# Attention, expert layer and gated layer on one core: the skipped TensorE code in loops, the tile table in two parts, w2's last pieces split in their own tile

## What is computed

```
state = f[t] * state + outer(k[t], v[t]);  y[t] = q[t] @ state      # B=4, H=8, S=768, D=48; f = sigmoid(f_logit)
x = y as 3072 tokens of 384
logits = x @ w_gate + modality_bias[modality_id];  e = argmax(logits)      # 8 experts
x = softmax(logits)[e] * (relu(x @ w1[e]) @ w2[e])                         # w1 384x1024, w2 1024x384
xn = x / sqrt(mean(x*x) + 1e-6) * rms_g
out = (silu(xn @ w_gate2) * (xn @ w_val)) @ w_out                          # 384x1536, 1536x384
```

## Time and profile before

| what | value |
|---|---|
| median of 3 runs | 838.8 us |
| lowest and highest | 836.85 and 844.91 us |
| the profiled execution | 838.23 us, span 836.5 us, mean TensorE clock 0.994 |
| TensorE matmuls | 811.1 us busy (97%) |
| TensorE weight loads | 737.0 us busy (88%) |
| VectorE | 452.0 us busy (54%) |
| ScalarE | 380.0 us busy (45%) |
| GpSimd | 140.5 us busy (17%) |
| DMA | 96.59 MB, mean 115 GB/s |

### The profile page before, as it was taken

One profiled execution on the slowest core, in us unless ns is written; L12 is line 12 of the kernel. 1 busy time (PEld: TensorE's weight loads), 2 busy tenths in 40 slices (PEclk: granted clock), 3 DMA queues, 4 the chain that ended last, 5 costly groups with the idle time before them and its releaser, 6 DMA issues.

```text
span 836.5 us, 15683 instructions
## 1 busy us (share of the span) xinstructions
PE 811.1 (97%) x5624; PEld 737.0 (88%) x5624; DVE 452.0 (54%) x715; ACT 380.0 (45%) x742; POOL 140.5 (17%) x170
## 2 busy tenths in 40 slices
PE   7999987799999999989999999999999999999997
PEld 6888877799999999988888888888988888888886
DVE  8989996886666666634433433333333334333331
ACT  6999975666665555534223312412332233122222
POOL 4003043785540000000001000200110010001001
...
GB/s 202 198 154 225 174 210 229 339 348 292 255 260 253 355 233 260 174 20 96 1 0 76 1 1 1 75 0 0 51 25 0 0 38 0 0 0 38 0 0 38
DMA packets 44121, 96.59 MB, mean 115 GB/s; under 512 B 9200, under 2 KB 25072, under 8 KB 43952
## 3 DMA queue, kind: packets, MB, share of 16 engines
...
q10 hardware_dynamic: 256, 0.79, 0.4%
...
HBM read 76.75 MB, written 19.29 MB: 115 GB/s over the span
## 4 chain that ended last, share of the span: by engine, by line
PE 88%; DVE 4%; issue 2%; ACT 2%; DMA 1%; POOL 0%; SPq 0%; DVEq 0%; ACTq 0%
PE h_ps L1887 16%; PE h_ps L1888 16%; PE h_ps L1886 16%; PE ym_ps L1886 7%; PE ym_ps L1888 7%; PE ym_ps L1887 7%; PE xTm_ps L1886 3%; PE xTm_ps L1888 3%; PE xTm_ps L1887 3%; PE sc_ps L839 2%; PE x_ps L859 2%; PE yT_ps L811 2%; PE ds_ps L783 1%; PE yT_ps L804 1%; PE turn_ps L830 1%
## 5 line engine op out<-in xcount | busy, mean ns | idle before, releaser
L1862 DVE TENSOR_TENSOR gs<-h_ps,sig 128x512 f32<-128x512 f32 x72 | 49.8, 692 | 177.2 <-ACT sig L1679 177.2
L1679 ACT ACTIVATE sig<-h_ps 128x512 f32<-128x512 f32 x72 | 43.1, 598 | 160.3 <-PE h_ps L1888 160.3
L1690 ACT CAST h_hi<-hid 128x512 fp32r<-128x512 f32 x72 | 44.6, 620 | 149.5 <-DVE hid L1865 149.5
L1886 PE MATMUL h_ps<-x_hi,w_hi 128*128 128x256 f32 x312 | 90.0, 289 | 8.4 <-DVE w_lo L271 4.5
L1887 PE MATMUL h_ps<-x_hi,w_lo 128*128 128x256 f32 x312 | 89.6, 287 | 0.0
L1888 PE MATMUL h_ps<-x_lo,w_hi 128*128 128x256 f32 x312 | 89.6, 287 | 0.0
L1888 PE MATMUL h_ps<-w_lo,wg_hi 128*128 128x512 f32 x216 | 85.2, 395 | 0.0
L1887 PE MATMUL h_ps<-w_hi,wg_lo 128*128 128x512 f32 x216 | 85.1, 394 | 0.0
L1886 PE MATMUL h_ps<-w_hi,wg_hi 128*128 128x512 f32 x216 | 84.1, 389 | 0.0
L1888 PE MATMUL h_ps<-w_lo,wv_hi 128*128 128x512 f32 x216 | 84.1, 389 | 0.0
L1886 PE MATMUL h_ps<-w_hi,wv_hi 128*128 128x512 f32 x216 | 84.0, 389 | 0.0
...
## 6 DMA issues: line engine op xcount, KB each, us to landing
...
```

The costliest lines, as they stand in the source:

```text
L1679: nc.scalar.activation(sig[:], g_ps, ACT.Sigmoid).then_inc(sig_done, 1)
L1690: nc.scalar.copy(h2_hi[:, fb % HELD], hid[:]).then_inc(h2_hi_done, 1)
L1862: nc.vector.tensor_tensor(gs[:], g_ps, sig[:], ALU.mult).then_inc(gs_done, 1)
L1886: nc.tensor.matmul(out, hi, rhs_hi, start=first, stop=False)
```

## The change

1. TensorE's part of general attention is put in loops: one copy of the body instead of eight. Rows are loaded a second time, into a buffer of their own (`rows_in`), for that.
2. The flag's reduction and comparison come one step sooner on VectorE, its matmul ahead of the read on TensorE. GpSimd doesn't wait for its scatters at the end of attention.
3. The tile table is written in two parts with one increment each: experts and ends of regions, then the rows, the number of tiles and the last tile. SyncE loads w1's first quarter of tile 1, pads, and loads the second after the first part; x of tile 1 after the second. `rt.count` moves behind `hidden(0)`; `rt.place` now stands ahead of `lo_w2(0, 0)`.
4. w2's pieces 2 and 3 are split in their own tile (after `h(0)` and `h(1)`), not in the tile before; in tile 0 all pieces of tile 0 are split between the h, `rows_of_tiles` and `gates_of_tokens` come at the end, and only pieces 0 and 1 of tile 1 are split there. GpSimd starts its thirds after piece 1 of tile 1.

```diff
@@ -570,11 +570,6 @@
-    for b in range(B):
-        pool.wait_ge(scattered[b], 16 * (LATE // B))
-    pool.wait_ge(scattered_late, 16 * B)
-    pool.wait_ge(ended, 16 * B)
-
 def scalar(act):
@@ -746,11 +741,11 @@
             first.lo_w1(nc, dve, 2, ahead_sems).then_inc(shared.w1_split, 1)
-        if at(c, CH) and b == 0:
-
+        if at(c, CH - 1) and b == B - 1:
             nc.vector.tensor_reduce(least[:], decay[:], AX.XY, ALU.min).then_inc(own_steps, 1)
...
             nc.vector.tensor_scalar(small[:], least[:], LEAST_DECAY, None, ALU.is_lt).then_inc(own_steps, 1)
+        if at(c, CH) and b == 0:
             first.lo_w1(nc, dve, 0, ahead_sems).then_inc(shared.w1_split, 1)
@@ -840,10 +835,10 @@
         if at(c, CH) and b == 1:
-            read(c, b, tile(c, b, 2))
             pe.wait_ge(marks, 2 * Routing.PLACED + Routing.CHOSEN + 2)
...
             nc.tensor.matmul(flag_ps, rt.ones_r[:], small[:], start=True, stop=True).then_inc(flag_sum, 1)
+            read(c, b, tile(c, b, 2))
             pe.wait_ge(ks_done, GROWN)
@@ -993,7 +989,8 @@
                 sp.wait_ge(tile_done, c * B + b + 1)
-                sp.dma_start(rt.x[:, LAST_SLOT + b, :], x_rows[c * B + b]).then_inc(tile_in, 16)
+                for rows in (rt.x[:, LAST_SLOT + b, :], rows_in[:]):
+                    sp.dma_start(rows, x_rows[c * B + b]).then_inc(tile_in, 16)
@@ -1131,22 +1128,21 @@
-        def group(c):
-            for b in range(B):
+        with pe.Fori(0, CH) as c:
+            with pe.Fori(0, B) as b:
                 n = c * B + b
-                pe.wait_ge(tile_in, n * 16 + 16)
+                pe.wait_ge(tile_in, n * 32 + 32)
                 for j in range(PR):
-                    mm = nc.tensor.transpose(pair_ps[:, j], rt.x[:, LAST_SLOT + b, 2 * D * j:2 * D * (j + 1)], ident[:])
+                    mm = nc.tensor.transpose(pair_ps[:, j], rows_in[:, 2 * D * j:2 * D * (j + 1)], ident[:])
                 mm.then_inc(pair_turned, 1)
...
                 mm.then_inc(lgt_done, 1)
-            if not is_last(c):
+            with pe.If(c < CH - 1):
                 pe.wait_ge(redone, c * Routing.PLACED + Routing.CHOSEN)
...
-        groups(pe, group)
         first.turn(nc, pe, xT_ps, ident, again)
@@ -1432,13 +1428,15 @@
             e1 = expert(1)
-            pad(e1)
             for g in range(GR):
+                sp.wait_ge(w1_split, g + 1)
+                load_w1(e1, g)
+                if g == 0:
+                    pad(e1)
                 if g == 1:
+                    sp.wait_ge(table_ready, 2)
                     sp.wait_ge(scattered, 16 * B)
                     load_x(1)
-                sp.wait_ge(w1_split, g + 1)
-                load_w1(e1, g)
             for g in range(GR):
@@ -1539,7 +1537,7 @@
     pool.wait_ge(made, 6)
-    pool.wait_ge(x_split, 2)
+    pool.wait_ge(w2_split, GR + 2)
     third_cols = F2 // KD
@@ -1605,8 +1604,7 @@
     act.wait_ge(shared.ahead.w2_landed, 16 * GR)
-    for g in range(GR):
-        hi_w2(0, g)
+    hi_w2(0, 0)
@@ -1619,20 +1617,30 @@
             if place != "last":
-                act.wait_ge(y_part, j * PARTS + (g + 1 if g < GR - 1 else PARTS))
+                act.wait_ge(y_part, j * PARTS + g + 1)
                 hi_w2(j + 1, g)
+
+        def own_w2(g):
+            if place != "first":
+                act.wait_ge(y_part, j * PARTS)
+            hi_w2(j, g)
...
         hi_h(0)
-        if place != "first":
+        if place == "first":
+            hi_w2(0, 1)
+        else:
+            own_w2(2)
             next_w1(0)
...
         if place == "first":
-            for i in range(EARLY):
-                hi_third(i)
+            own_w2(2)
+            own_w2(3)
+            hi_third(0)
         else:
+            own_w2(3)
             next_w1(1)
@@ -1656,14 +1664,14 @@
             next_w2(0)
-            next_w2(1)
-        next_w2(2)
         for s in range(SUB):
...
             nc.scalar.copy(y_kept_rows[:, s], y_ps[:, s, 0:DM]).then_inc(y_kept, 1)
-        next_w2(3)
+        if place == "first":
+            next_w2(1)
+            hi_third(1)
         if place == "middle":
@@ -1722,24 +1731,25 @@
         link(nc.vector.tensor_tensor_scan(tiles_to[:], ones_e[:], n_tiles[:], 1.0, ALU.mult, ALU.add))
-
-    def table_of_tiles():
         link(nc.vector.tensor_tensor(past[:], tile_no[:].rearrange("p (t o) -> p t o", o=1).broadcast_to([P, MT, E]),
                                      per_tile(tiles_to[:]), ALU.is_ge))
-        nc.vector.tensor_reduce(entries[:, 0:MT], past[:], AX.X, ALU.add)
+        link(nc.vector.tensor_reduce(entries[:, 0:MT], past[:], AX.X, ALU.add))
+        nc.vector.tensor_scalar(table[:, BEHIND:BEHIND + E], rt.base[:], 1.0, None, ALU.add)
+        nc.vector.tensor_scalar(table[:, 0:MT], entries[:, 0:MT], float(E - 1), None, ALU.min).then_inc(table_ready, 1)
+
+    def table_of_tiles():
+
         link(nc.vector.tensor_tensor(skipped[:], past[:], per_tile(gain[:]), ALU.mult))
...
         nc.vector.tensor_scalar(is_first[:], entries[:, 0:MT], first.expert_f[:, 0:1], float(TM), ALU.is_equal, ALU.mult)
+        nc.vector.memset(entries[:, MT:FIRST], float(E - 1))
         link(nc.vector.scalar_tensor_tensor(entries[:, FIRST:FIRST + MT], tile_no[:], float(TM),
                                             entries[:, FIRST:FIRST + MT], ALU.mult, ALU.add))
-        nc.vector.tensor_scalar(entries[:, 0:MT], entries[:, 0:MT], float(E - 1), None, ALU.min)
-        nc.vector.memset(entries[:, MT:FIRST], float(E - 1))
-        nc.vector.scalar_tensor_tensor(entries[:, FIRST:FIRST + MT], is_first[:], -float(TM), entries[:, FIRST:FIRST + MT],
-                                       ALU.add, ALU.add)
-        nc.vector.tensor_scalar(entries[:, BEHIND:BEHIND + E], rt.base[:], 1.0, None, ALU.add)
-        nc.vector.tensor_scalar(entries[:, LAST:LAST + 1], tiles_to[:, E - 1:E], -1.0, None, ALU.add)
-        link(nc.vector.tensor_copy(entries[:, USED:USED + 1], tiles_to[:, E - 1:E]))
-        nc.vector.tensor_copy(table[:], entries[:]).then_inc(table_ready, 1)
+        nc.vector.tensor_scalar(table[:, LAST:LAST + 1], tiles_to[:, E - 1:E], -1.0, None, ALU.add)
+        nc.vector.tensor_copy(table[:, USED:USED + 1], tiles_to[:, E - 1:E])
+        link(nc.vector.scalar_tensor_tensor(entries[:, FIRST:FIRST + MT], is_first[:], -float(TM),
+                                            entries[:, FIRST:FIRST + MT], ALU.add, ALU.add))
+        nc.vector.tensor_copy(table[:, MT:BEHIND], entries[:, MT:BEHIND]).then_inc(table_ready, 1)
@@ -1790,9 +1800,9 @@
     first.lo_w1(nc, dve, GR - 1, shared.ahead).then_inc(w1_split, 1)
-    lo_w2(0, 0)
     dve.wait_ge(counted, 1)
     rt.place(nc, dve, CH - 1, B, (CH - 1) * B, pre_ps, cnt_ps, marks, 0)
+    lo_w2(0, 0)
@@ -1808,18 +1818,19 @@
+        lo_h(0)
         if place == "first":
             tiles_of_experts()
-        lo_h(0)
-        if place == "first":
-            table_of_tiles()
         else:
+            lo_w2(j, 2)
             next_w1(0)
...
             shifted_scores()
-            lo_w2(0, 2)
+            table_of_tiles()
+        else:
+            lo_w2(j, 3)
         if place == "last":
@@ -1828,15 +1839,14 @@
         if place == "first":
+            lo_w2(0, 2)
             lo_w2(0, 3)
-            rows_of_tiles()
             next_w1(0)
...
         if place == "first":
-            gates_of_tokens()
             next_w1(1)
@@ -1847,9 +1857,9 @@
             next_w2(0)
+            rows_of_tiles()
+            gates_of_tokens()
             next_w2(1)
-        next_w2(2)
-        next_w2(3)
@@ -1909,9 +1919,6 @@
             for i in range(2):
-                if place == "first" and g == 0 and i == 1:
-                    pe.wait_ge(marks, Routing.CHOSEN)
-                    rt.count(nc, B, pre_ps, cnt_ps).then_inc(counted, 1)
                 cols = slice(i * P, (i + 1) * P)
@@ -1932,6 +1939,9 @@
         hidden(0)
+        if place == "first":
+            pe.wait_ge(marks, Routing.CHOSEN)
+            rt.count(nc, B, pre_ps, cnt_ps).then_inc(counted, 1)
         hidden(1)
...
```

6 lines of the change are left out of this document (4 added, 2 removed).

## The result

The changed kernel takes 852.46 us (median of 6 runs, 851.48 to 853.17) beside 840.19 of the kernel before in the same comparison (836.85 to 844.91): ratio 1.014, 95% interval 1.011 to 1.017. It is slower by 1.4%, and lies outside the predicted range of 830 to 844.5. The profiled execution took 851.78 us around a span of 850.0: 13.5 more than the span of before. Of these 13.5, 1.8 lie ahead of the experts: attention's last turn of `x_ahead` came at 130.0 us here and at 128.2 before.

What follows compares the result with a forecast made beforehand. TensorE is busy nearly all of the span, so only some 11 us of idle or slow stretches can be won. Terms -4.0 - 1.8 + 1.4 + 1.6 + 0.6 + 0.2 = -2.0 take 838.8 to 836.8 us, range 830 to 844.5.

Steps and rivals of the forecast that it cites:

- Term 4: Tiles 2 to 11: moving w2's last pieces delays the x load to T+8.9, with no slack left; +1.4 us (0 to +8).
- term 5: Tiles 1 and 2: GpSimd's later chain delays SyncE's loads for tile 3, w1 late at ScalarE; +1.6 us (0 to +5).
- rival C: Every tile's turn waits for the late x load; a 5 us landing makes 1.1 a tile, 846.4 us; chance 0.2.
- term 1: Start of tile 0: shorter skip avoids the late instruction block; TensorE starts at 131.3 instead of 135.6, at full clock.
- term 3: Inside tile 1: fewer `lo_w2` ahead of `lo_h(0)` shrink the hole from 2.7 to 1.0; -1.8 us (0 to -3).
- Term 2: Table in two parts: tile 1's x load leaves 3.5 us earlier, tile 1 starts at 154.1; -4.0 us (0 to -5.5).
- Term 6: Last tile: the load of y lands later, its squares put `hi_h(0)` later than TensorE needs; +0.6 us (0 to +2).
- B: Before tile 0: the block fetch stays or another replaces it, TensorE isn't brought forward; 841.6 us; chance 0.12.
- D: Loads land sooner, neither turn nor GpSimd's chain costs, tile 1's start gains its bound of -5.5; 831.7 us; chance 0.18.

Runs made afterwards that it cites:

- e9: Changed kernel with GpSimd's splits of the thirds cut to 16 of 512 columns, all loads kept: one run, 838.52 us beside 838.5.
- e5: Changed kernel with the gated layer's thirds and the load of wo three tiles later: 853.92 us, ratio 1.020 to the kernel before.
- the control: The kernel before, unchanged, profiled once more: 840.64 us.
- e7: Kernel before, with SyncE's x load held until VectorE has split h's third piece, all splits where they were: 861.24 us, ratio 1.028.
- e3b: Changed kernel with the next tile's x load issued ahead of the loads of w2's pieces 2 and 3: 838.4 us, ratio 0.999 to before.
- e1: Changed kernel with the splits of w2's pieces 2 and 3 put back into the tile before: 844.17 us, ratio 0.999 to before.
- e4: Kernel before with only the edits ahead of the experts (loops, tile of its own, flag's place): 845.72 us, ratio 0.999.
- e6: Changed kernel with GpSimd's first third waiting only for x of tile 1, as in the kernel before: one run, 848.62 us beside 838.79.
- e8: e3b with the later thirds and wo loaded behind the reload of a tile's weights on SyncE: 833.49 us, ratio 0.994 to before.

## Why the prediction failed

**Term 4 is the step that failed.** It gave +1.4 us for the x load in tiles 2 to 11; from the turn in tile 1 to the turn in tile 8 the changed kernel's first profile has 15.2 too many. These 15.2 hold what term 5 gave for tile 2, too (+1.6 forecast, 3.1 measured), so together 3.0 were forecast. The whole comes out by stretches, changed against before, each in its first profile: -4.1 to the start of tile 1, -0.1 to its turn, +15.0 from there to the last turn and +0.9 behind it, which makes 11.7, and 1.8 of attention ahead of them. Term 4's mechanism was right: rival C, with a chance of 0.2. The position was right too: in an undisturbed tile the load leaves 3.9 us ahead of the turn, which is T+8.9 as computed. What the term lacked:

- *The worst tiles instead of the median one.* The chain `lo_w2(j,3)`, load, x load was put together from VectorE's 0.95 per split. In the tiles with GpSimd at work up to two of the splits in this chain take 1.45 to 2.05 us. The row was in the prediction: four `lo_w2` at 1.46 each beside GpSimd. It was used for term 5, in tile 2, and not for term 4. Before the change 4.6 us of slack swallowed it; the change spent that slack, and e9 shows that without the slow splits the turns of the x of tiles 3 to 6 have 0.25 at most. The Trainium skill (SBUF — State Buffer, section "SBUF: two separate sides") says that such a VectorE operation and a GpSimd operation exclude each other for a whole instruction. The trace agrees that one waits for the other, in the timeline of the changed kernel: one split took 5.18 us, in place of 0.95, and ended 0.8 behind the last of GpSimd's three subtractions. It was held for all three, though its record begins before theirs: longer than one instruction of the other. This split delayed no turn: the x load had left at 187.67. The prediction had that rule and asked only what it would make of one tile.

```profile
188.09 5.18 DVE L1777 TENSOR_TENSOR w_lo<-w_raw,w_hi 128x768 fp32r<-128x768 f32 x1
...
188.69 3.76 POOL L1546 TENSOR_TENSOR wg_lo<-g_in,wg_hi 128x512 fp32r<-128x512 f32 x3
```

- *The clock.* Each hole was priced at its own length. Three of them had 3.4 us at half clock with them, 1.7 us lost each time, a third of the loss. The fall at 133.5 in the earlier trace rows was read and used for term 1 only.
- *A load behind a large one.* Tile 9's hole (1.23) comes with wo's load: it moved with it in e5. It and tile 2's are made by a quarter of w1 that lands late. The prediction's chain has no such wait, though the profile of before shows that load in tile 1 under way for 9.1 us (156.32 to 165.43).
- *Two landings.* The sum of 1.4 has ten of the twelve landings. The two left out are those of tiles 1 and 2, 4.2 and 6.6 us, the longest of all among them. Tile 2's turn was put down to term 3, which has nothing for it; there the hole of 1.89 stood.

The landings themselves were shorter than feared: 3.3 to 4.5 us, median 3.4 and not 4.0, none of 6.6. Rival C's 1.1 us a tile over ten tiles came nearer (846.4) by luck, from a uniform landing of 5 us.

**Term 1** (tile 0 brought forward by the shorter skip). TensorE started right behind `x_lo` (131.73 plus 0.96, first matmul 132.74), the clock stayed up, the waits behind it were 1.03 and 0.66 where 1.0 and 0.8 were given. But the base was one execution. The same stretch A took 29.9, 28.6 and 27.4 in three profiles of the same code (the second is the control, the third e7 with a hole of 2.82); where attention ends late the fetch is covered. The 4.46 us were the largest of the three, not the usual. What the loops themselves give can only be seen where attention ends early: the old code had 4.46 and 2.82 before tile 0 then (in e7 the q8 packet moved at 131.7, 2.8 ahead of the start, as 2.7 in the earlier trace rows), and the new code had no hole in any of six profiles with the last turn of `x_ahead` between 128.8 and 130.3. So the hole does go with the loops, though no run has them alone with an early end.

**Term 2** (tile 1 sooner). Forecast: tile 1 starts 25.9 us behind the last turn of `x_ahead` (154.1 less 128.2); it was 25.7 and 26.4. The gain was 4.2 against the first profile of before, and 1.0 to 2.9 for either of the changed kernel's profiles against the other two. Inside, the first table came as computed (141.57, 11.6 behind that turn, for 11.9), the x load 18.2 behind it for 17.1, since the pad landed in 4.4 us and not in 2.8.

**Term 3** (inside tile 1, -1.8): from tile 1's first matmul to its turn it took 15.8 us before and 15.8 after, with a new hole of 1.89 before the turn. Without that it is 13.9 (e3b: 13.9), -1.9. But the base varies: the hole was 2.70 in the first profile of before, 2.56 in e7 and 2.84 in e1, and only 0.74 in the control, which has 14.6 for the stretch, and 1.08 in e4.

**Term 5** (GpSimd's and SyncE's later start, +1.6). e6 takes back GpSimd's start and gains 2.0; e8, which keeps SyncE from waiting for it, gains 6.2 over e3b in the sum, 5.8 in B. The chain was the one described (SyncE ahead of the loads for tile 3, w1 late before `hi_h(1)`); its size in e3b was 2.71 plus the clock. In the changed kernel itself it didn't bind: ScalarE waited 0.59 us for that load, beside a VectorE that was in a slow split (1.68 us) until then. Tile 2's 3.1 us are its hole of 1.31 and the half clock that came with tile 1's.

**Term 6** (last tile, +0.6): from the last turn to the gated layer's first turn it took 22.98 us (362.97 to 385.95), and 22.04 before (350.38, the turn 17.6 us behind the one at 332.78, to 372.42): +0.9. ScalarE waited 5.06 us for the load of y ahead of the squares, as described.

**The rivals.** B and D did not happen: tile 0 came forward, and the turns cost. C's condition, more than 0.34 us a tile, was met more than fourfold.
